# Regrouping transposed probabilities between partitions: half through DRAM, or all of it by direct SBUF transfers issued from two engines

## What is computed

```python
kv_pool = kv.reshape(B, H // 4, 4, W // 4, 4, C).mean(axis=(2, 4))   # B = 2, H = 384, W = 32, C = 128
k = v = kv_pool.reshape(B, -1, C) @ w_sr                             # 768 keys a batch
s = (q @ k.transpose(0, 2, 1)) / np.sqrt(C)                          # q: 2 x 12288 x 128
a = np.exp(s - s.max(-1, keepdims=True))
x = (a / (a.sum(-1, keepdims=True) + 1e-9)) @ v
h = x @ w_in;  x = (h * np.cos(h)) @ w_out                           # 128 -> 2048 -> 128
h = x @ w2_in; y = (h / (1 + np.exp(-1.702 * h))) @ w2_out           # 128 -> 2048 -> 128
```

## Time and profile before

| | |
|---|---|
| median of 3 runs | 2647.89 us (2643.92 to 2653.43) |
| the profiled execution | 2649.51 us |
| its span, first to last instruction | 2647.8 us |
| busy: PE, ACT, DVE, POOL | 98%, 71%, 78%, 82% |
| granted clock of TensorE, mean | 0.993 |
| DMA: bytes moved, mean rate | 193.89 MB, 73 GB/s |
| DMA busy, first eight of 40 slices (66 us each), in tenths | 7, 9, 9, 9, 8, 9, 9, 9 |
| read from and written to DRAM | 92.34 and 63.01 MB |

### The profile page before, as it was taken

One profiled execution on the slowest core, in us unless ns is written; L12 is line 12 of the kernel. 1 busy time (PEld: TensorE's weight loads), 2 busy tenths in 40 slices (PEclk: granted clock), 3 DMA queues, 4 the chain that ended last, 5 costly groups with the idle time before them and its releaser, 6 DMA issues.

```text
span 2647.8 us, 37678 instructions
## 1 busy us (share of the span) xinstructions
PE 2587.5 (98%) x11797; PEld 2136.3 (81%) x11797; DVE 2068.8 (78%) x2264; ACT 1880.8 (71%) x2280; POOL 2173.4 (82%) x1830
## 2 busy tenths in 40 slices
PE   8998989889999999999999999999999999999999
PEld 6787777768888888888888888888888888888887
DVE  8777777777878787777777777787778777787876
ACT  4666766677777777777777777777777777777776
POOL 2777889789888888888888888888888888888883
PEclk9999999999999999999999999999999999999999
DMA  7999899920000000101000101010000000101000
GB/s 258 313 296 294 273 281 292 279 93 21 12 24 12 23 20 16 24 12 24 12 24 12 24 12 24 12 24 12 24 12 24 12 24 12 24 12 24 17 12 13
DMA packets 191147, 193.89 MB, mean 73 GB/s; under 512 B 113456, under 2 KB 138352, under 8 KB 190064
## 3 DMA queue, kind: packets, MB, share of 16 engines
q1 hardware_dynamic: 176208, 155.28, 20.7%
q10 hardware_dynamic: 14880, 37.89, 4.1%
HBM read 92.34 MB, written 63.01 MB: 59 GB/s over the span
## 4 chain that ended last, share of the span: by engine, by line
PE 85%; DMA 7%; SPq 3%; POOL 3%; DVE 1%; issue 1%; ACT 0%; POOLq 0%
PE psum L685 27%; PE psum L687 27%; PE psum L686 27%; SPq L469 2%; DMA q_blocks<-in_q 2%; DMA bounce<-turned 2%; POOL probs_t_lo L595 1%; DMA gathered<-bounce 1%; POOL g_lo L670 1%; PE psum L757 1%; PE psum L759 1%; PE psum L769 1%; DVE neg_max L1268 1%; DMA bounce<-turned_last 1%; PE psum L787 1%
## 5 line engine op out<-in xcount | busy, mean ns | idle before, releaser
L670 POOL TENSOR_TENSOR g_lo<-g,g_hi 128x512 fp32r<-128x512 f32 x768 | 1126.6, 1467 | 66.8 <-ACT g_hi L1183 6.7
L1401 DVE TENSOR_TENSOR g_lo<-g,g_hi 128x1024 fp32r<-128x1024 f32 (+1 forms) x396 | 643.8, 1626 | 434.6 <-ACT g L1178 433.1
L1176 ACT ACTIVATE g_hi<-psum 128x1024 fp32r<-128x1024 f32 (+1 forms) x396 | 397.3, 1003 | 558.7 <-PE psum L687 558.7
L667 POOL CAST g_hi<-g 128x512 fp32r<-128x512 f32 x750 | 558.4, 745 | 226.5 <-DVE g L1392 226.5
L685 PE MATMUL psum<-x_hi,w_lo 128*128 128x512 f32 x1536 | 598.0, 389 | 0.8 <-DVE g L1392 0.8
L685 PE MATMUL psum<-g_hi,w_lo 128*128 128x512 f32 x1536 | 597.9, 389 | 0.8 <-POOL g_lo L670 0.8
L687 PE MATMUL psum<-x_hi,w_hi 128*128 128x512 f32 x1536 | 597.6, 389 | 0.0
L686 PE MATMUL psum<-x_lo,w_hi 128*128 128x512 f32 x1536 | 597.6, 389 | 0.0
L687 PE MATMUL psum<-g_hi,w_hi 128*128 128x512 f32 x1536 | 597.5, 389 | 0.0
L686 PE MATMUL psum<-g_lo,w_hi 128*128 128x512 f32 x1536 | 597.5, 389 | 0.0
L1392 DVE TENSOR_TENSOR g<-psum,g 128x512 f32<-128x512 f32 x768 | 490.3, 678 | 1.9 <-ACT g L1169 1.8
(11 more groups left out here) (87 smaller groups left out, 2483.4 us busy)
## 6 DMA issues: line engine op xcount, KB each, us to landing
gathered<-bounce SPq DMA_DIRECT2D x48, 768.0 KB, 5.5
gathered<-turned SPq DMA_DIRECT2D x256, 96.0 KB, 4.5
bounce<-turned ACTq DMA_DIRECT2D x64, 384.0 KB, 6.4
bounce<-turned_last ACTq DMA_DIRECT2D x32, 384.0 KB, 6.2
gathered<-turned_last SPq DMA_DIRECT2D x128, 96.0 KB, 4.7
x_dram<-x_out SPq DMA_DIRECT2D x48, 256.0 KB, 5.4
x_raw<-x_dram SPq DMA_DIRECT2D x48, 256.0 KB, 2.7
x_inv<-inverse_dram SPq DMA_DIRECT2D x48, 256.0 KB, 3.4
```

The lines of the kernel that those rows point to most:

```text
L667: nc.gpsimd.tensor_copy(g1_hi[at][:, t], g1[at][:, t]).then_inc(g1_hi_ready, 1)
L670: nc.gpsimd.tensor_tensor(g1_lo[at][:, t], g1[at][:, t], g1_hi[at][:, t].bitcast(F32), ALU.subtract).then_inc(g1_lo_ready, 1)
L1176: nc.scalar.activation(g2_hi[ring2(j, p)][:, t], h2[buffer2(j)][:, t], ACT.Silu, scale=GELU)
L1401: nc.vector.tensor_tensor(g2_lo[ring2(j, p)][:, t], g2[ring2(j, p)][:, t], g2_hi[ring2(j, p)][:, t].bitcast(F32), ALU.subtract).then_inc(g ...
```

## The change

The DRAM way is gone, with `bounce` and its semaphores. All sixteen blocks of a chunk are moved directly. Ten are issued by SP in `regroup(c)`, which no longer waits for anything between them, and six by ScalarE, one at a time, in three slots: in the slot with s % 4 == 3 one behind the exponential, one behind the rounding of queries (L1021) and one behind the copy of x1 (L1058); in the next slot one behind the exponential and one behind a rounding of probabilities; in the one after that one behind the exponential. For the last chunk they stand in the code written out behind the loop. Before its first one ScalarE waits for the four turned tiles, for the values of chunk c - 3 (whose buffer is written again) and, at one chunk, for a key piece; SP has the same waits as before. `regrouped[n]` now counts sixteen DMAs a chunk.

```diff
-    DIRECT = GROUPS // 2
-    REGROUPED = (DIRECT * GROUPS + 1) * 16
-    BOUNCED = (GROUPS - DIRECT) * 16
+    MOVES = [(a, f) for a in range(GROUPS) for f in range(GROUPS)]
+    BY_SP, BY_ACT = MOVES[:10], MOVES[10:]
+    REGROUPED = len(MOVES) * 16
...
-                for a in range(DIRECT):
-                    for f in range(GROUPS):
-                        sp.dma_start(flat(dst[f * BLK:(f + 1) * BLK, a]),
-                                     flat(src[a * BLK:(a + 1) * BLK, f])
-                                     ).then_inc(regrouped[n], 16)
-                sp.wait_ge(bounced[n], BOUNCED * (c // 3 + 1))
-                sp.dma_start(dst[:, DIRECT:GROUPS].rearrange("p a k t -> p (a k t)"),
-                             bounce[c].rearrange("f p x -> (f p) x")
-                             ).then_inc(regrouped[n], 16)
+                for a, f in BY_SP:
+                    sp.dma_start(flat(dst[f * BLK:(f + 1) * BLK, a]),
+                                 flat(src[a * BLK:(a + 1) * BLK, f])
+                                 ).then_inc(regrouped[n], 16)
...
-            def bounce_groups(c):
+            def regroup(c, m):
 
                 b, n = c // CB, c % 3
-                act.wait_ge(turned_made, (c + 1) * SUB)
-                for a in range(DIRECT, GROUPS):
-                    at = slice((a - DIRECT) * KEYS, (a - DIRECT + 1) * KEYS)
-                    src = turned[b][n][a * BLK:(a + 1) * BLK, :, :, :]
-                    nc.scalar.dma_start(
-                        bounce[c][:, :, at].rearrange("f p x -> p f x"),
-                        src.rearrange("p f k t -> p f (k t)")
-                    ).then_inc(bounced[n], 16)
+                if m == 0:
+                    act.wait_ge(turned_made, (c + 1) * SUB)
+                    if c >= 3:
+                        act.wait_ge(values_summed, c - 2)
+                    if c == CB + 1:
+                        act.wait_ge(piece_made, 4)
+                a, f = BY_ACT[m]
+                nc.scalar.dma_start(flat(gathered[b][n][f * BLK:(f + 1) * BLK, a]),
+                                    flat(turned[b][n][a * BLK:(a + 1) * BLK, f])
+                                    ).then_inc(regrouped[n], 16)
...
             for s in range(TILES - 1):
                 if s + 2 < TILES:
                     exponentials(s + 2)
-                if s % SUB == SUB - 1:
-                    bounce_groups(s // SUB)
+                chunk, phase = divmod(s + 1, SUB)
+                if phase == 0:
+                    regroup(chunk - 1, 0)
+                elif phase < 3 and chunk >= 1:
+                    regroup(chunk - 1, 2 * phase + 1)
                 c, i = divmod(s - HI_SLOT, SUB)
                 if c >= 0 and i < (BY_POOL if c < CHUNKS - 2 else PARTS):
                     round_probabilities(c, i)
+                if phase == 1 and chunk >= 1:
+                    regroup(chunk - 1, 4)
                 if s % SUB == 1:
                     guard_totals(s // SUB)
                 if (s + 5) % SUB == 0 and 2 <= (s + 5) // SUB < CHUNKS:
                     split_queries((s + 5) // SUB, q_ps)
+                if phase == 0:
+                    regroup(chunk - 1, 1)
                 if s >= STORE_SLOT and (s - STORE_SLOT) % SUB == 0:
                     store_x1((s - STORE_SLOT) // SUB)
+                if phase == 0:
+                    regroup(chunk - 1, 2)
...
-            bounce_groups(CHUNKS - 1)
+            regroup(CHUNKS - 1, 0)
             store_x1(CHUNKS - 4)
+            regroup(CHUNKS - 1, 1)
             nc.scalar.activation(silu_probe[:, :], half_pi[:, :], ACT.Silu)
+            regroup(CHUNKS - 1, 2)
             round_probabilities(CHUNKS - 2, 0)
+            regroup(CHUNKS - 1, 3)
+            regroup(CHUNKS - 1, 4)
             count_turns(0, 0)
+            regroup(CHUNKS - 1, 5)
```

More of the change, by code:

```diff
@@ L233, in attention_and_networks @@
     x1_dram = nc.dram_tensor("x1_dram", (CHUNKS, P, TOK), F32, kind="Internal").ap()
-    bounce = nc.dram_tensor("bounce", (CHUNKS, GROUPS, BLK, (GROUPS - DIRECT) * KEYS), F32,
-                            kind="Internal").ap()
     inverse_dram = nc.dram_tensor("inverse_dram", (CHUNKS, TOK), F32, kind="Internal").ap()
@@ L323, in attention_and_networks @@
     turned_made = sem("turned_made")
-    bounced = [sem(f"bounced{n}") for n in range(3)]
     regrouped = [sem(f"regrouped{n}") for n in range(3)]
```

## The result

| | before | after |
|---|---|---|
| median | 2648.44 us (4 runs, 2643.92 to 2653.43) | 2605.88 us (4 runs, 2603.66 to 2607.92) |
| span of the profiled execution | 2647.8 us | 2605.0 us |
| mean granted clock | 0.993 | 0.998 |
| moved by DMA | 193.89 MB | 156.17 MB |
| read from and written to DRAM | 92.34, 63.01 MB | 54.59, 25.26 MB |

The ratio of the times is 0.9839, with a 95% interval of 0.9819 to 0.9859: 42.6 us less, 1.6%. The range held it, the direction was right, and the gain was a third larger than the 31 us of the forecast.

What follows compares the result with a forecast made beforehand. Stalls from SP and busy DMA engines, and the slower clock behind them, held chunks above TensorE's pace. Gains of 24 us (211.8 to 520.1 us), 4 (before) and 3 (tail) made 31, giving 2617 us; range 2596 to 2655.

Steps and rivals of the forecast that it cites:

- The bound: Attention chunks if only TensorE set them: 8.90 us, 10.69 with pooling; 155.9 us for 48.7 to 211.8, 259 for 211.8 to 520.1.
- The cause: SP's long direct issues (eight take 8.20 us) come from a full queue in front of DMA engines 92% busy.
- SP: Its turn per chunk, ten direct transfers and three others, falls from about 10.1 to 7.6 to 8.5 us, below 8.90.
- ScalarE: Its six issues per chunk, each behind another instruction, cost nothing, at most 0.6 us; uncovered they would cost 3.6 us.
- Direct transfers: At 309 GB/s per busy time a chunk needs 7.2 us of DMA engine time (bounds 7.0 and 9.1), share 0.75 to 0.8.
- GpSimd: In 16 chunks where it also splits weights it needs 9.54 us against 8.90, adding 10 us.
- The weight places: Three places where weight loads stand in SP's queue ahead of direct issues: 4 us left for each, 12 us.
- The jitter of 3: A guessed 3 us added to the forecast for 211.8 to 520.1 us, which came to 284 us.
- The first stretch: 48.7 to 211.8 us, 15 attention chunks, 163.1 us measured, 7 over its bound: 4 us taken back.
- The shared issue path: Rival: SP and ScalarE share a stage passing all sixteen transfers singly, 11.3 us a chunk, about 2689 us; chance 0.15.
- The ports: Rival: direct transfers need 9.1 us of engine time a chunk, about 2631 us; chance 0.19 together with half the gain.
- ScalarE held by its issues: Rival: two of ScalarE's six issues run long, 3 us a chunk ahead of exponentials, some 2648 us; chance 0.08.

Runs made afterwards that it cites:

- Experiments 1 to 3: Kernel before, one part changed each: read without waiting for the writes, 2641.57 us; fewer bytes through DRAM, 2610.69 us; four direct transfers moved to ScalarE, 2680.05 us.
- experiment 4: Kernel after, but all sixteen direct transfers issued by SP: 2723.95 us.
- experiment 6: Kernel after, but ScalarE's six issues in one block behind the exponential of the slot with s % 4 == 3: 2672.99 us.
- 7: Kernel after, but ScalarE's six issues in one block behind the rounding of queries and the copy of x1: 2634.68 us.
- experiment 8: Kernel after, block order changed so that SP and ScalarE more often read from the same half of the partitions: 2609.69 us.
- experiment 3: Kernel before, but four of SP's eight direct transfers issued by ScalarE, same bytes and hop: 2680.05 us.
- experiment 11: Kernel after, plus one unneeded 384 KB write per chunk from SBUF to DRAM, issued by SP ahead of its ten: 2646.21 us.

## Why the prediction was right, and where it was off

The main step was right: the bytes, through the busy DMA engines, made the stalls, and without them a chunk goes at TensorE's or GpSimd's pace. Some terms of the sum were off, and part of the good fit of the rest is errors that cancel.

**The bound.** A chunk of 8.90 or 10.69 us by TensorE was right: the first stretch took 153.8 us against the 155.9 worked out.

**The cause.** I read SP's long issues as a full queue ahead of busy engines. Experiments 1 to 3 bear it out: the wait was worth 7 us, the bytes 38, and the issues without the bytes cost 32. What I didn't see is that the parts don't add up. Moving issues off SP with the bytes still there cost time; with the bytes gone it is worth 118 us (experiment 4).

**SP.** Its turn was put at 7.6 to 8.5 us; by the lines above it is 6.30 + 0.28 + 0.35 + 0.39 and gaps, 7.5; with the longer issues and the weight loads in other chunks the mean from 210 to 480 us is some 8.3.

**ScalarE.** Six issues at nothing was right, and the cover that I named is what makes it so: in one block, mostly uncovered, they cost 67 us (experiment 6) or 29 (7). I had written 3.6 us a chunk for that, but no time for the kernel. Multiplied out over 44 chunks it would have been 158, too much; a part of it is taken up by ScalarE's idle time.

**Direct transfers.** I had expected a DMA share near 0.75 to 0.8 and it is 0.86. Taken at 309 GB/s per busy time, the transfers came slower: 278.5 x 0.86 / 29 = 8.3 us of engine time a chunk instead of 7.2, inside my bounds of 7.0 and 9.1. By the same split as before, 1.57 MB in 8.3 - 2.2 = 6.1 us, 258 GB/s. That is above the 200 that I had estimated from the Trainium skill (SBUF — State Buffer, "Door 1: The DMA port swizzle"), whose figures are for one transfer at a time, which no run here has; which half is read made no difference (experiment 8). It didn't move the time, since 8.3 still fits into 8.90.

**GpSimd.** 9.54 us in the chunks with weight splits, measured 9.55. 15 chunks show it, 9.9 us against my 10.

**The weight places.** This is the term that was mis-sized. I left 4 us for each of three, 12 in all. The first cost 3.3 us of stall and 2.0 in the next chunk, partly at the slower clock (0.91 granted from 234 to 246 us), the other two nothing. At those SP has one load in its queue and not two, and where it otherwise stands some 2 us a chunk for others, it hardly does from 342 to 368 us: it makes up in that time. The jitter of 3 was a guess, and a handover of keys at chunk 23 that costs some 4 us in both kernels had been left out. Together 284 expected; measured 259 + 9.9 + 5.3 + 4.3 = 278.5, with no jitter left over. Here 6.7 us too much for the loads and 3 for jitter are partly hidden by the 4.3 left out.

**The first stretch.** I took 4 of 7 us back and it was 9.3. Two chunks in it lie partly in gaps of the pooling, so its bound was lower than mine, and the pieces of rows disturbed nothing. The forecast lacked 5.3 us here, 5.5 in the second stretch and 0.7 outside of both (3.7 against 3), together nearly the 11.6 us by which the gain is larger than 31.

**The rivals.** The shared issue path is ruled out for transfers of this kind: beside six of ScalarE's at a median of 0.51 us, SP's take a median of 0.60, as in the kernel before, and from 312.00 us all sixteen go out in 6.4 us, 0.40 each, under the 0.58 from which that rival decides. The ports are answered above: 8.3 us of engine time, not 9.1. ScalarE held by its issues is no rival of this kernel but the outcome of experiment 3. The other side, slower, came in experiments 3, 4 and 6, each with one part of the change undone or moved.

## What to carry to other kernels

When a queue's issues turn long, look first at what the DMA engines have to move, and take bytes away before spreading issues over more queues. Issues on a computing engine were free here one at a time, each beside an instruction about as long. As a block they held up the instruction behind them, for 2.0 to 2.9 us a chunk, and it cost more than twice as much where other engines waited for that instruction (67 us against 29). Leave the issuing engine some time to stand in each turn: without it, every extra transfer in its queue becomes a stall. For a change made of parts, test each part alone: here one gives 1.4%, one 0.3% and one costs 1.2%.

## What the runs showed of the hardware that I had not expected

- Issue times of DMAs lengthen at a mean DMA share of 0.89 (7.88 instead of 6.30 us for ten, experiment 11), and on either engine, also on the one whose own queue got nothing more: 23 of ScalarE's 155 issues over 1 us there, 3 of 168 without the write.
- Undisturbed, a direct transfer of 96 KB takes its engine 0.51 to 0.60 us to issue, on SP as on ScalarE at the same time, while a save of 256 KB takes 0.35.
- A subtraction of 128 x 512 on VectorE with both inputs in SBUF took 2.65 us beside GpSimd's, twice GpSimd's own 1.30, and 0.69 where GpSimd stood still.
- Two thirds of a megabyte a chunk of plain traffic and 1.57 MB of direct transfers between 32 partitions each keep the engines busy for 8.3 us, 272 GB/s by busy share, against 309 before.
